# One level of Strassen's seven products in the feed-forward stages of a fused attention and feed-forward kernel

## The reference

```python
kv  = einsum('bhsd,bhse->bhde', k, v)            # 8 batches, 8 heads, 576 rows, 64 wide
o   = einsum('bhsd,bhde->bhse', q, kv)
x   = o / sqrt(mean(o*o, -1) + 1e-6) * g_norm    # reshaped to 4608 tokens x 512
u   = sigmoid(x @ w_gate) * (x @ w_val)          # 512 -> 1536, twice
x   = u @ w_mid                                  # 1536 -> 512   (moe_w_out)
h   = x @ w_in                                   # 512 -> 2048
g   = where(h > 0, h, exp(min(h, 0)) - 1)
out = g @ w_out                                  # 2048 -> 512, all float32
```

## Time and profile before

| | us |
|---|---|
| median of three runs (lowest, highest) | 1837.48 (1836.17, 1838.25) |
| the profiled execution, whole | 1837.31 |
| its span in the trace | 1835.5 |
| PE busy (98% of the span) | 1807.7 |
| PE weight loads busy | 1504.7 |
| DVE, ACT, POOL busy | 741.7, 387.8, 81.9 |

### The profile page before, as it was taken

The page is one execution under the profiler, slowest core; times in us unless marked ns, Lnnn a source line. Parts: engine busy times, 40 slices in busy tenths (PEclk is TensorE's granted clock), DMA queues, the critical chain, the costliest instruction groups (busy, mean ns, idle before and its releaser), DMA issues.

```text
span 1835.5 us, 21760 instructions
## 1 busy us (share of the span) xinstructions
PE 1807.7 (98%) x8304; PEld 1504.7 (82%) x8304; DVE 741.7 (40%) x1240; ACT 387.8 (21%) x710; POOL 81.9 (4%) x117
## 2 busy tenths in 40 slices
PE   7998999999999999999999999999999999999999
PEld 6887888888888888888888888888888888888887
DVE  3676532222222222212222376454545454444443
ACT  6784310101111010101010232121212121211111
POOL 3552000000000000000000000000000000000000
PEclk9999999999999999999999999999999999999999
DMA  9895420000101010101010132010101010101000
GB/s 235 246 277 184 131 75 1 32 14 2 44 0 46 0 46 0 46 0 46 0 46 0 59 124 69 1 46 0 46 0 46 0 46 0 46 0 46 1 22 23
DMA packets 69792, 93.74 MB, mean 51 GB/s; under 512 B 4736, under 2 KB 43648, under 8 KB 69760
## 3 DMA queue, kind: packets, MB, share of 16 engines
q1 hardware_dynamic: 69232, 92.29, 16.6%
q10 hardware_dynamic: 528, 1.05, 0.2%
HBM read 65.01 MB, written 28.31 MB: 51 GB/s over the span
## 4 chain that ended last, share of the span: by engine, by line
PE 90%; DMA 1%; DVE 1%; issue 0%; ACT 0%; POOL 0%; SPq 0%; POOLq 0%; ACTq 0%; DVEq 0%
PE bank L470 53%; PE bank L487 37%; DMA qkv<-in_k_dram 0%; DMA w_raw<-in_moe_w_in_dram 0%; DVE o L681 0%; ACT y L627 0%; POOL sq L393 0%; PE bank L420 0%; DMA x_gated<-y 0%; DMA out_dram<-y 0%; PE bank L438 0%; PE bank L429 0%; DVE w_pre L701 0%; DVE x_hl L695 0%; PE bank L439 0%
## 5 line engine op out<-in xcount | busy, mean ns | idle before, releaser
L470 PE MATMUL bank<-x_hl,w_rest 128*128 128x512 f32 x3024 | 713.2, 389 | 0.0
L470 PEld LDWEIGHTS bank<-x_hl,w_rest 128*128 128x128 f32 x3024 | 567.8, 188 | 117.7
L487 PE MATMUL bank<-w_rest,u_hl 128*128 128x512 f32 x1620 | 386.3, 389 | 0.8 <-DVE u_hl L712 0.8
L487 PEld LDWEIGHTS bank<-w_rest,u_hl 128*128 128x128 f32 x1620 | 304.0, 188 | 64.2 <-issue 1.2
L719 DVE TENSOR_TENSOR u_f<-bank,act_f 128x512 f32<-128x512 f32 x108 | 74.7, 691 | 618.9 <-PE bank L470 618.9
L470 PE MATMUL bank<-x_hl,w_pre 128*128 128x512 f32 x1296 | 302.3, 389 | 2.0 <-DVE x_hl L695 1.3
L470 PEld LDWEIGHTS bank<-x_hl,w_pre 128*128 128x128 f32 x1296 | 243.0, 188 | 53.4 <-DVE x_hl L695 2.2
L487 PE MATMUL bank<-u_hl,w_rest 128*128 128x512 f32 x1188 | 282.4, 389 | 0.0
L487 PEld LDWEIGHTS bank<-u_hl,w_rest 128*128 128x128 f32 x1188 | 223.0, 188 | 46.2
L613 ACT ACTIVATE act_f<-act_f 128x512 f32<-128x512 f32 x144 | 91.0, 632 | 591.8 <-DVE act_f L733 591.8
L733 DVE TENSOR_SCALAR act_f<-bank 128x512 f32<-128x512 f32 x144 | 99.4, 690 | 270.4 <-PE bank L470 270.4
(11 more groups left out here) (50 smaller groups left out, 666.2 us busy)
## 6 DMA issues: line engine op xcount, KB each, us to landing
qkv<-in_q_dram SPq DMA_DIRECT2D x32, 288.0 KB, 5.2
qkv<-in_k_dram SPq DMA_DIRECT2D x32, 288.0 KB, 5.7
qkv<-in_v_dram SPq DMA_DIRECT2D x32, 288.0 KB, 6.1
x_attention<-o SPq DMA_DIRECT2D x32, 288.0 KB, 3.6
x_gated<-y SPq DMA_DIRECT2D x36, 256.0 KB, 2.0
x_raw<-x_gated SPq DMA_DIRECT2D x9, 1024.0 KB, 5.2
out_dram<-y SPq DMA_DIRECT2D x36, 256.0 KB, 2.0
x_raw<-x_attention SPq DMA_DIRECT2D x8, 1024.0 KB, 5.2
```

The source lines that it names most:

```text
L470: mm = pe.matmul(dst[:, :], w[:, a, m * P:(m + 1) * P], x_hl[:, m, b, :], start=(m == 0 and a == b == 0), stop=(m == KT - 1 and a == 1))
L487: mm = pe.matmul(ACC[m][:, :], lhs, rhs, start=(j == 0 and a == b == 0), stop=(j == tiles - 1 and a == 1))
```

## The change

Each large product C = A x B becomes one level of the Strassen-Winograd scheme: tokens, inner and output features are halved, giving quarters, and seven half-size products take the place of eight. Four sums of quarters of the activations (`S1` to `S4`) and four of the weights come first. The seven are issued in the order P1, P2, P6, P5, P7, P3, P4; P6, P7 and P4 add onto P1's PSUM accumulator, P3 onto P5's. On the way ACT copies the accumulator out after P1, P6 and P5 (a snapshot), and DVE adds P2, P7 and P3's results to the snapshots (`combine`): the quarters 11, 22, 12 of the output. Quarter 21 is what is left in the accumulator after P4.

The stages no longer run together. There are four phases, each over all tokens, with the hidden values going through DRAM as float32 (`u_gated`, 1536 x 4608, and `u_elu`, 2048 x 4608):

- Phase 1, gated: 36 units (12 visits to six super-blocks of 768 tokens, first one half of the hidden features, then the other, three units each). A unit is 7 products of 12 matmuls, 128x384 moving.
- Phase 2, `w_mid`: 6 units of 7 products of 36 matmuls, 384 columns.
- Phase 3, elu: 24 units (six super-blocks, four units each) of 7 products of 12 matmuls, 384 columns.
- Phase 4, `w_out`: 18 units of 256 tokens, 7 products of 24 matmuls, 256 columns.

Weights come in 17 chunks. POOL makes their sums, ACT and DVE split the seven items of a chunk. Chunks 0 to 2 go straight to their places in SBUF. The 14 others are split through two small buffers (`out_w`), stored item by item (512 KB each) in DRAM (`weight_items`), and loaded when their phase nears. The splitting of a chunk is spread over a phase 1 unit, one item per product: units 0, 1, 3, 4, 6, 7, 9, 10, 12, 13, 15, 21, 22, 24, 25 and 27 carry chunks 1 to 16. Units that carry none split x for the next visit if they are last of their visit; the sums of x are made in the middle unit of each visit. The parts of the diff that matter, cut:

```diff
+    MID, IN, OUT = UNITS1, UNITS1 + 3, UNITS1 + 7
+    CHUNKS = UNITS1 + 11
+    DIRECT = 3
+    CHUNK_UNIT = {1: 0, 2: 1, 3: 3, 4: 4, 5: 6, 6: 7, 7: 9, 8: 10, 9: 12, 10: 13, 11: 15,
+                  12: 21, 13: 22, 14: 24, 15: 25, 16: 27}
```

SP's list, in phase 1:

```diff
+            for n in range(FIRST2):
+                vis, j = n // HALF1, n % HALF1
+                if j == 0 and vis + 1 < VISITS1:
+                    sp.wait_ge(s_lo, split1(vis, P4))
+                    load_x(x1_dram, (vis + 1) % NS)
+                for c, at in ((2, 0), (3, 1), (4, 3), (5, 4), (6, 6), (7, 7), (8, 9), (9, 10), (10, 12), (11, 13),
+                              (12, 18), (13, 19), (14, 22), (15, 24), (16, 25)):
+                    if n == at:
...
+                        load_chunk(c)
+                if n == unit1(NS - 1, 1):
...
+                    load_unit(3, BUF1[3])
+                    sp.wait_ge(s_prod, prod(n - 1, P4))
+                    load_unit(4, BUF1[4])
...
+                for i in (0, 1):
+                    store_weight(n, i)
+                store_gated(n, "11")
+                for i in (2, 3, 4):
+                    store_weight(n, i)
+                store_gated(n, "22")
+                store_weight(n, 5)
+                store_gated(n, "12")
+                store_weight(n, 6)
+                store_gated(n, "21")
```

SP's list, in phase 3 and at the start of phase 4:

```diff
+                if vis + 1 == NS and j > 0:
+                    sp.wait_ge(s_prod, prod(n - 1, P4))
+                    load_out_cells(BUF3[j - 1])
+                for c in NAMES:
+                    store_elu(n, c)
+            load_out_cells(BUF3[3])
+
+            load_raw4(1)
```

POOL, the sums of a chunk's quarters:

```diff
+            def weight_sums(c):
+                t1, t2 = (by_item(staging(c)[1][:, n, :], c) for n in range(2))
+                b11, b12, b21, b22 = (quarter(c, kh, fh) for kh in range(2) for fh in range(2))
+                if c >= 1:
+                    pool.wait_ge(s_wlo, ITEMS * (c - 1) + P5 + 1)
+                pool.wait_ge(s_wraw[c % 2], raw_loaded(c))
+                pool.tensor_tensor(t1, b12, b11, ALU.subtract).then_inc(s_wsum, 1)
+                pool.tensor_tensor(b12, b22, b12, ALU.subtract).then_inc(s_wsum, 1)
+                pool.wait_ge(s_wsum, 4 * c + 1)
+                pool.tensor_tensor(t2, b22, t1, ALU.subtract).then_inc(s_wsum, 1)
+                pool.wait_ge(s_wsum, 4 * c + 3)
+                pool.wait_ge(s_wlo, ITEMS * c + P2 + 1)
+                pool.tensor_tensor(b21, b21, t2, ALU.subtract).then_inc(s_wsum, 1)
```

PE, what each product waits for:

```diff
+            def wait_target(n, i):
+                if i == P1 and n >= 2:
+                    pe.wait_ge(*c21_taken(n - 2))
+                if i == P2 and n >= 1:
+                    pe.wait_ge(s_comb, comb(n - 1, "11"))
+                if i == P6:
+                    pe.wait_ge(s_snap, snap(n, P1))
+                if i == P5 and n >= 1:
+                    pe.wait_ge(s_comb, comb(n - 1, "12"))
+                if i == P7:
+                    pe.wait_ge(s_snap, snap(n, P6))
+                if i == P3:
+                    pe.wait_ge(s_snap, snap(n, P5))
+                if i == P4:
+                    pe.wait_ge(s_comb, comb(n, "22"))
```

ACT, the rounding of a chunk's item and a unit of phase 1:

```diff
+            def split_weight(c, i):
+                if c >= DIRECT and stored(c, i) >= 2:
+                    act.wait_ge(s_wst[stored(c, i) % 2], 16 * (stored(c, i) // 2))
...
+                act.activation(weight_split(c, i, 0), weight_item(c, i), ACT.Copy).then_inc(s_whi, 1)
...
+            def gated_unit(n):
+                pa = PA[n % 2]
+                fill1(n, 0)
+                act.wait_ge(s_prod, prod(n, P1))
+                wait_count(act, s_u, comb(n - 1, "11"))
+                act.activation(s1[:, :, :], pa[:, :, 0:NT], ACT.Copy).then_inc(s_snap, 1)
+                fill1(n, 1)
+                act.wait_ge(s_comb, comb(n, "11"))
+                act.activation(s1[:, 0, :], s1[:, 0, :], ACT.Sigmoid).then_inc(s_sig, 1)
+                fill1(n, 2)
+                act.wait_ge(s_prod, prod(n, P6))
+                wait_count(act, s_u, comb(n - 1, "12"))
+                act.activation(s2[:, :, :], pa[:, :, 0:NT], ACT.Copy).then_inc(s_snap, 1)
+                fill1(n, 3)
+                act.wait_ge(s_prod, prod(n, P5))
+                act.activation(s5[:, :, :], PB[:, :, 0:NT], ACT.Copy).then_inc(s_snap, 1)
+                fill1(n, 4)
+                act.wait_ge(s_comb, comb(n, "22"))
+                act.activation(s5[:, 0, :], s5[:, 0, :], ACT.Sigmoid).then_inc(s_sig, 1)
```

DVE, the same unit (`fill1` splits an item's low part, or makes a sum of x):

```diff
+                fill1(n, 0)
+                combine(n, "11", s1[:, :, :], PC[:, :, 0:NT])
+                fill1(n, 1)
+                gate("11", 0, s1)
+                fill1(n, 2)
+                fill1(n, 3)
+                combine(n, "22", s5[:, :, :], pa[:, :, 0:NT])
+                fill1(n, 4)
+                gate("22", 1, s5)
+                combine(n, "12", s2[:, :, :], PB[:, :, 0:NT])
+                fill1(n, 5)
+                gate("12", 2, s2)
+                fill1(n, 6)
```

DVE, from a unit of phase 3 (the exponentials between `minimum` and `result` are ACT's):

```diff
+                fill3(n, 3)
+                combine(n, "22", s5[:, :, :], pa[:, :, 0:NT])
+                minimum("22", e1, s5)
+                fill3(n, 4)
+                result(1, e1, s5)
+                combine(n, "12", s2[:, :, :], PB[:, :, 0:NT])
+                minimum("12", e0, s2)
+                fill3(n, 5)
+                result(2, e0, s2)
+                fill3(n, 6)
```

DVE, from a unit of phase 4, the sums of the next 256 tokens:

```diff
+                    name = {1: "S3", 2: "S2", 4: "S1", 6: "S4"}.get(i)
+                    if name and vis + 1 < NR:
+                        sum_u2(vis + 1, name)
```

More of the change, by code:

```diff
@@ L50, in build @@
     RING = 2 * NP
-    assert T % NT == 0 and S == SP_ * RT and D == 64 and DM == NT
+    QR = 4
+    QK = 4
+    assert S == SP_ * RT and D == 64 and (T, DM, F1, F2) == (4608, 512, 1536, 2048)
+    ITEMS = 7
+    P1, P2, P6, P5, P7, P3, P4 = range(ITEMS)
+    NT = 384
+    SUPER = 2 * NT
+    NS = T // SUPER
+    TT = 128
+    NR = T // (2 * TT)
+    UNITS1 = F1 // 256
+    HALF1 = UNITS1 // 2
+    VISITS1 = 2 * NS
+    UNITS3 = F2 // 512
+    FIRST2 = VISITS1 * HALF1
+    FIRST3 = FIRST2 + NS
@@ L63, in build @@
[L63 to L106, removed]
+        def view(stack, tensors):
+            at, made = 0, []
+            for name, shape, dt, start in tensors:
+                if start > at:
+                    stack.enter_context(nc.sbuf_tensor(f"gap_{name}", [P, (start - at) // 4], F32))
+                assert start >= at
+                made.append(stack.enter_context(nc.sbuf_tensor(name, shape, dt)))
+                size = 4
+                for n in shape[1:]:
+                    size *= n
+                at = start + -(-size // 32) * 32
+            return made
@@ L164, in col_tile @@
[L164 to L183, removed]
-        place = {(kind, j): s for kind, j, s, _ in first_use}
-        order = {(kind, j): n for n, (kind, j, _, _) in enumerate(first_use)}
-        def weights_at(into, onto, j):
-            keys = [(kind, j + LEAD + 1) for kind in into] + [(onto, j + 1)]
-            return [order[x] for x in keys if x in order]
@@ L193, in build, with c21_taken @@
-        AHEAD1 = list(range(PRE))
-        AHEAD2 = list(range(N_GATED, order[("out", 0)] + 1))
-        assert AHEAD1[-1] == order[("mid", 0)] and len(AHEAD2) <= WR
+        s_u = sem("s_gated_result")
+        s_e = sem("s_elu_result")
+        s_c21 = [sem(f"s_c21_taken{n}") for n in range(1, 5)]
+        s_st = [sem(f"s_result_stored_{c}") for c in ("11", "22", "12", "21")]
+        def c21_taken(n):
+            for phase, first in ((3, FIRST4), (2, FIRST3), (1, FIRST2), (0, 0)):
+                if n >= first:
+                    return s_c21[phase], n - first + 1
@@ new lines, in out_item, with slot4, mid_cell, out_cell @@
+        def out_item(vis, i):
+            raw = raw4[vis % 2]
+            a11, a12, a21, a22 = (raw[:, kh:kh + 8, th:th + TT] for th in (0, TT) for kh in (0, 8))
+            return {P1: a11, P2: a12, P6: sum_4[:, :, :], P5: a11, P7: a21, P3: a12, P4: a22}[i]
+        def slot4(vis, i):
+            return (5 + ITEMS * vis + i) % 6
+        def mid_cell(i, t):
+            return 3 * i + t
+        def out_cell(i, c):
+            return (21 + 4 * i + c) % 28
+        def tokens(sup, th):
+            return slice(sup * SUPER + th * NT, sup * SUPER + (th + 1) * NT)
@@ L515, in elu_block, with target @@
[L515 to L526 removed]
+            def target(n, i):
+                return {P2: PC, P5: PB, P3: PB}.get(i, PA[n % 2])
@@ new lines, in hidden_product @@
+            def hidden_product(n, i, cell, slot):
+                dst, w = target(n, i), wreg[:, cell]
+                for g in range(2):
+                    for kt in range(2):
+                        cols = slice((2 * g + kt) * P, (2 * g + kt + 1) * P)
+                        for a, b in PARTS:
+                            mm = pe.matmul(dst[:, g, 0:NT], w[:, a, cols], ring[:, slot, b, kt, :],
+                                           start=(i in STARTS and kt == a == b == 0),
```

(2 more changed lines are left out.)

1119 lines of the change are left out of this document (839 added, 280 removed).

## The result

The changed kernel takes 1813.59 us in the median of four runs (1811.93 to 1816.53); the kernel before takes 1837.57, also in the median of four; the ratio is 0.987, with a 95% interval of 0.9855 to 0.9889. The forecast was 1869 us, 1.7% slower. The profiled execution took 1814.1 us, with a span of 1812.3.

What follows compares the result with a forecast made beforehand. Before the change only PE's stream of columns was taken to count. With everything hidden 172.7 + 1498.4 = 1671.1 us; adding 136 + 14 + 6 + 4 + 18 + 13 + 3 + 4 gave 1869 us, range 1775 to 1935.

Steps and rivals of the forecast that it cites:

- PE stream: All phases: 6552 matmuls of 384 columns at 173.3 ns and 3024 of 256 at 120 ns, 1498.4 us, 166.2 less.
- phase 1 beyond its stream: Phase 1: 136 us for visits slowed by DVE, stores and queue, 6 for units 16 to 18, 4 for the clock.
- phase 3: Elu units: a chain of 8.1 to 9.3 us against PE's 8.32, splits at block ends; +18 us (5 to 40).
- visit 0: Phase 1's first visit, without stores: 8.5 us lost to DVE's 42.9 us of work and half of GpSimd's.
- The rival of the 188 ns weight load: Every matmul paced by its weight load at 188 ns: 172.7 + 1800 + stalls, over 2000 us; chance 0.02.
- the width of a weight item: Phase 1 items priced at 1024 columns: 1.22 us per DVE low part, 2.3 us per GpSimd subtraction, DVE 42.9 us a visit.
- The first two mechanisms: Phase 1 visits: GpSimd holding up DVE, 18.3 us at most; stores with two buffers, 5.3 us per two items against PE's 4.16.
- the same walk: Three engines' lists through a two-chunk visit: 37 + 14.6 + about 5 = 56 to 57 us, plus 5 for GpSimd: 62.
- The queue: Visit start: x and the raw chunk ahead of the first store, 8.3 us; third item some 6.5 us late.
- The rival at 1925: Gaps at P7, P3 and P4 bring PE's 1.2 GHz clock, costing 58 us: about 1925 us; chance 0.17.
- the second, 1801: Phase 1: the GpSimd lock or the stores, not both in series, a visit near 52 us: 1801 us; chance 0.20.
- The sign of being wrong: The forecast is wrong if visits 1 to 4 last under 50 us, or the clock falls through phase 1.

Runs made afterwards that it cites:

- e7: Changed kernel with GpSimd's four subtractions per chunk cut to 8 columns and two of seven weight items rounded from a plain quarter: 1813.5 us, ratio 0.986.
- e1: Changed kernel with only the places in SP's list moved at which raw weight chunks are loaded, seven into units that store none: 1778.2 us, ratio 0.968.
- e5: Changed kernel with ACT and DVE doing each item of chunks 1 to 16 twice, and four more GpSimd subtractions per chunk from 2: 1902.6 us, ratio 1.036.
- e6: Changed kernel with useless matmuls ahead of P7, 36 in a visit's first unit and 16 in its second, in 14 units: 1816.1 us, ratio 0.988.
- e8: Changed kernel with the edits of e1 and e4 together, four item buffers and early raw chunks: 1726.9 us, ratio 0.939.
- e4: Changed kernel with four buffers for the split weight items and not two, loads left where they were: 1744.5 us, ratio 0.949.
- e3: Changed kernel with the raw chunk moves of e1, and x for the next visit loaded behind the third weight item's store: 1775.9 us, ratio 0.967.

## Why the prediction was wrong

Its terms against the trace, in us. The PE stream per stage is the count of matmuls times 173.3 or 120 ns; what a stage takes beyond is read from the first and last matmul of its line (179.72 is P6 of unit 0, phase 1 to 800.8, phase 2 to 1062.9, phase 3 to 1432.4, phase 4 to 1809.7). With the 172.7 us kept from before, the measured terms make the 1814.1 of the profiled execution.

| term | forecast | measured |
|---|---|---|
| PE stream | 1498.4 | 1498.5 |
| start | +14 | +11.3 |
| phase 1 beyond its stream | +146 (136, 6, and 4 for the clock) | +101.1 |
| phase 2 | +4 | 0 |
| phase 3 | +18 | +20.1 |
| border to and phase 4 | +16 | +14.4 |
| end behind the last matmul | 0 | -4.0 |

45 of the 55 us that the forecast was too slow are in phase 1. There the six visits with stores take 55.4 to 57.4 us where 62 was forecast (33 us in all), and visit 0 and the others the rest.

- **The PE stream** was right. The rival of the 188 ns weight load falls. The agreement of 173.3 and 120 to the last digit is partly chance: 0.66 us for five matmuls in the earlier trace rows is 132 ns and was rounded to 133; with 132 the same line gives 172.6 and 118.5, 9 us less in all.
- **The step that failed is the width of a weight item**: "7 x 1.22 = 8.5 more" for DVE and "four subtractions of 1024 columns per chunk" for GpSimd. A quarter of a chunk is 512 columns: the raw chunk has 2048 in four quarters. The 1024 in the shape of `weight_items` are its high and low part. The prediction's own 512 KB for an item say so: 128 partitions x 2 parts x 512 columns x 4 bytes; 1024 columns would be 1 MB. So DVE had, at the prediction's prices, 35.5 us of work in a visit of 43.7 and not 42.9 (34.2 measured), and two items' round trip was 0.63 + 0.69 + 2.7 + 0.2 = 4.2 us and not 5.3. The first two mechanisms cost nothing here: e7 takes GpSimd away and gains nothing, and in e1 the second unit's stop goes with the round trip as it was. Repriced afterwards, with 29 + 14.6 + 9 = 53 for a visit, the same walk gives 9 x 6 and some 13 for units 15 and 27, about 67 in place of 136, so 1800: faster, and 14 below the measurement. That it comes so near is partly luck: its phase 1 is 24 us too short, its other terms 10 too long. By this sum the factor of two decides the sign. e5 agrees in direction, 1902.6 and slower, with more work than the width would add.
- **GpSimd**: the hold of the earlier trace rows is in the new trace (0.74 us for 0.69 on low parts, 0.63 for 0.56 on gates), but e7 shows that it cost nothing, against the 5 us a visit in the forecast.
- **The queue**: right in place and kind, and it carried the loss. In the visit from 292.45 to 349.84, 57.4 us, 10.2 are stops and 3.5 slower matmuls. The walk had the third item 6.5 us late in the first unit and 2 to 3 in the middle one, but counted only 5 of that beyond the round trip. Its 56 to 57 us before GpSimd is near the measured 57.4 by luck: a round trip too long by 1.1 us for two items stood where more waiting for the queue and the slower matmuls were. x was priced at 315 GB/s, 5 us; its loads take 6.6 in the median. That x and the chunk add up was wrong (e1).
- **Visit 0** had no stop at all in the changed kernel behind that of its start, for lack of stores; 8.5 were forecast.
- **The clock**: it fell as the earlier trace rows suggested, and e6 shows that the 31 us it seems to cost were covered. The rival at 1925 falls.
- **Phase 3**: 60.1 us a block of four units against 58.2, where the forecast had 3 us a block; DVE's minimum runs at 560 ns, the lower of the two prices. The first 360 matmuls take 8 us more than their stream, behind stores of x and u of 14.8 and 12.5 us with weight loads ahead of them, which I hadn't named there, and the last 312 take 5 more. The sum of 18 was right partly by that.
- **The rival nearest to what came** was the second, 1801, held at 0.20. It had the lock or the stores alone, and e7 and e8 show that it was the stores; its visit near 52 us was too short against 57.4, and the other terms made up for it.
- **Small slips**: the line for DVE through 692 and 460 ns has 162 ns at no columns and not 157; the prices read from it, 0.56, 0.96 and 1.22 us, hold. The sign of being wrong, "visits 1 to 4 last under 50 us", didn't come, though the forecast was wrong; what spoke against it were the low parts of items, 0.69 and 0.74 us in the means of their two groups and not over 1.22.

## What to carry to other kernels

Before pricing a step, count its elements from the access pattern, and once more from the bytes it moves, where one factor decides the sum: here the width decided whether DVE had time to spare, and an item's 512 KB would have given it away. The round trip through DRAM with room for two was paced here by the loads ahead of its store; more room (e4, 69 us) beat reordering the loads (e3, 38 us). And idle time or a lower clock of an engine is a symptom until an experiment that removes it alone moves the time (e6 did not).

## What the runs showed of the hardware

- Matmuls with a new 128x128 weight load each follow at 120.1, 173.3 and 226.7 ns for 256, 384 and 512 columns: 0.417 ns a column and 13.3 ns, though each weight load is recorded at 188 to 193 ns.
- A 512 KB store took 2.7 us in the median of 98. The first of a visit took 8.5 to 10.2, with x (1.57 MB), or x and a raw chunk (2.6 MB together), issued just before it from the same engine; behind x alone in e1 it took 8.5.
- PE's granted clock was 0.91 to 0.94 in the stretches of phase 1 with stops of 3.1 to 7.1 us, between its two levels of 1.2 and 2.4 GHz: 84 matmuls behind the longer stops took 16.2 to 17.8 us, and not 14.6. It was 0.97 to 1.00 when useless matmuls filled the stops (e6). After the stops of 1.4 to 2.2 us in e4, 84 took 14.8 to 14.9, and after one of 1.9 us in e6 16.4, so the length of a stop alone doesn't tell.
- GpSimd took 1.28 to 1.29 us for a subtraction of 512 columns in runs of 128 while DVE stood (three in a row from 293.74), and 1.44 to 1.61 in the means of its four groups, most of them with DVE at work. DVE's minimum over 768 columns in SBUF took 560 ns, its two-input operations of that width 958.
